# A three-stage attention-and-experts kernel: the two small score stages of neighbouring units put into common steps, and both units prepared one tile ahead

## The reference, cut to what matters

```python
def _attn_ref(q, k, v, alpha):                   # q, k, v, alpha: (4, 8, 768, 48)
    state = np.zeros((B, H, D, D))
    for t in range(S):
        state = alpha[:, :, t, :, None] * state + np.einsum('bhd,bhe->bhde', k[:, :, t], v[:, :, t])
        y[:, :, t] = np.einsum('bhd,bhde->bhe', q[:, :, t], state)
    return y

def _moe_ref(x, w_in, w_out):                    # x: (3072, 384), d_ff 2048
    h = x @ w_in
    g = np.where(h > 0.0, h, np.exp(np.minimum(h, 0.0)) - 1.0)
    return g @ w_out

def _moe2_ref(x, domain_probs, w1, w2):          # 4 experts, 1024 wide
    p = domain_probs / (domain_probs.sum(-1, keepdims=True) + 1e-09)
    for e in range(E):
        out += p[:, e:e + 1] * (np.maximum(x @ w1[e], 0.0) @ w2[e])
    return out

# reference: y = attention; x = y as (3072 tokens, 384); moe2(moe(x))
```

## Time and profile before

| what | value |
|---|---|
| time, median of 3 runs | 1290.7 us |
| the profiled execution, its time and its span | 1291.18 us, 1289.4 us |
| TensorE (PE) busy | 1276.2 us, 99% of the span |
| VectorE (DVE) busy | 849.3 us, 66% |
| ScalarE (ACT) busy | 631.6 us, 49% |
| GpSimd (POOL) busy | 500.3 us, 39% |
| granted TensorE clock | full in all 40 slices |

### The profile page before, as it was taken

How to read it: one execution, slowest core, us unless ns; L and a number is a source line. 1 busy time by engine, 2 the same in 40 slices (tenths; PEclk the granted TensorE clock), 3 DMA queues, 4 the chain that set the end, 5 groups by cost and what they waited for, 6 DMA issues and landing times.

```text
span 1289.4 us, 24688 instructions
## 1 busy us (share of the span) xinstructions
PE 1276.2 (99%) x9681; PEld 1055.8 (82%) x9681; DVE 849.3 (66%) x1245; ACT 631.6 (49%) x1051; POOL 500.3 (39%) x416
## 2 busy tenths in 40 slices
PE   7999999999999999999999999999999999999999
PEld 7888888888888888888888888888888888888887
DVE  8777868665676765676766567676567555654445
ACT  2766444367434357634436743435763444653332
POOL 2147959510476720084752056671009300000011
PEclk9999999999999999999999999999999999999999
DMA  4354635463445245436336344534543333523330
GB/s 174 105 200 131 191 120 167 128 176 108 163 147 164 87 116 167 142 130 208 103 107 175 123 141 149 158 99 129 153 161 111 98 100 98 156 86 111 98 98 26
DMA packets 84343, 170.92 MB, mean 133 GB/s; under 512 B 29186, under 2 KB 30722, under 8 KB 84228
## 3 DMA queue, kind: packets, MB, share of 16 engines
q1 hardware_dynamic: 83936, 169.21, 42.6%
q10 hardware_dynamic: 292, 0.14, 0.0%
HBM read 163.24 MB, written 6.08 MB: 131 GB/s over the span
## 4 chain that ended last, share of the span: by engine, by line
PE 97%; DVE 1%; issue 0%; DMA 0%; ACT 0%; SPq 0%; DVEq 0%; ACTq 0%
PE ps_o L699 16%; PE ps_h L699 15%; PE ps_o L701 15%; PE ps_o L700 15%; PE ps_h L701 15%; PE ps_h L700 15%; PE ps_att L677 1%; PE ps_att L603 1%; PE ps_att L635 1%; PE ps_att L520 1%; PE ps_att L534 1%; DMA alpha<-in_a 0%; DVE k_level L835 0%; DVE q_low L834 0%; DVE blocks L858 0%
## 5 line engine op out<-in xcount | busy, mean ns | idle before, releaser
L899 DVE TENSOR_TENSOR w_lo<-w_stage,w_hi 128x768 fp32r<-128x768 f32 x288 | 332.5, 1155 | 33.9 <-ACT w_hi L1125 30.5
L699 PE MATMUL ps_o<-g_hi,w_lo 128*128 128x512 f32 x864 | 341.1, 395 | 0.0
L701 PE MATMUL ps_o<-g_hi,w_hi 128*128 128x512 f32 x864 | 336.5, 389 | 0.0
L700 PE MATMUL ps_o<-g_lo,w_hi 128*128 128x512 f32 x864 | 336.4, 389 | 0.0
L699 PE MATMUL ps_h<-x_hi,w_lo 128*128 128x512 f32 (+1 forms) x861 | 335.3, 389 | 0.2 <-DVE x_lo L939 0.2
L701 PE MATMUL ps_h<-x_hi,w_hi 128*128 128x512 f32 (+1 forms) x861 | 334.5, 389 | 0.0
L700 PE MATMUL ps_h<-x_lo,w_hi 128*128 128x512 f32 (+1 forms) x861 | 334.5, 389 | 0.0
L1156 ACT ACTIVATE g_hi<-ps_h 128x512 fp32r<-128x512 f32 x184 | 110.0, 598 | 432.3 <-PE ps_h L701 432.3
L919 DVE SCALAR_TENSOR_TENSOR g_lo<-ps_h,g_hi 128x512 fp32r<-128x512 f32 x184 | 126.7, 689 | 207.9 <-ACT g_hi L1156 207.8
L1125 ACT CAST w_hi<-w_stage 128x768 fp32r<-128x768 f32 x288 | 239.3, 832 | 8.6 <-DMA w_stage<-in_w 7.3
L330 POOL TENSOR_TENSOR products<-blocks 128x384 f32<-128x384 f32 x150 | 191.4, 1295 | 94.3 <-DMA blocks<-in_a_blocks 71.5
(11 more groups left out here) (115 smaller groups left out, 943.9 us busy)
## 6 DMA issues: line engine op xcount, KB each, us to landing
w_stage<-in_w SPq DMA_DIRECT2D x288, 384.0 KB, 3.2
k_level<-in_k SPq DMA_DIRECT2D x12, 512.0 KB, 6.1
q_low<-in_q SPq DMA_DIRECT2D x12, 512.0 KB, 6.9
alpha<-in_a SPq DMA_DIRECT2D x12, 512.0 KB, 4.0
v_tok<-in_v SPq DMA_DIRECT2D x12, 512.0 KB, 4.5
p_rows<-p_norm SPq DMA_DIRECT2D x6, 1024.0 KB, 9.0
values_states<-in_v_heads SPq DMA_DIRECT2D x20, 256.0 KB, 4.6
out<-acc SPq DMA_DIRECT2D x18, 256.0 KB, 4.3
```

The lines of the kernel that those rows point to most:

```text
L699: nc.tensor.matmul(dst, lhs[1], rhs[0], start=first, stop=False)
L700: nc.tensor.matmul(dst, lhs[0], rhs[1], start=False, stop=False)
L701: return nc.tensor.matmul(dst, lhs[0], rhs[0], start=False, stop=last)
L899: nc.vector.tensor_tensor(wl[n % WRING][:], stage[n % STAGE][:], wh[n % WRING][:].bitcast(F32), ALU.subtract).then_inc(w_low, 1)
```

## The change: what it does

1. **Common pieces.** Both units of a tile begin their pieces at the same step (4; in tile 0, 15), and `PIECES` is now a pair of tables, one for even and one for odd units. Levels 16 and 32 of the odd unit fall into the same steps as those of the even one (piece 0 and 2). The later pieces of the odd unit come at 13, 15 and 23. In level 16 and 32 the even unit uses the left half of the bank and the odd unit the right half (`level_bank`).
2. **Put aside.** ScalarE copies the odd unit's scores from PSUM to `scores_aside` (`set_aside`, three copies of 128x256), and places them from there when the even unit's attention is done.
3. **Both units prepared ahead.** The odd unit's `unit`, `blocks`, `low` and `block` jobs move from steps 12 to 28 of its own tile into the tile in front. `PARTS_AT` has three columns now: tile 0, tile 1, and tiles 2 and up.
4. **Waits.** `bank_free` is replaced by functions that name the reader of each bank. The load of the queries waits for the placing of those of two units back.
5. **Last sums.** The last two steps' outputs are made sum by sum, the third in two halves of 256 tokens in the `ps_att` banks, and added and stored in four parts (`LAST_SUMS`, `last_outputs`, `add_last`).

```diff
-PIECES = {0: ("L", LOW), 2: ("L", LOW + 1), 4: ("K", 0), 6: ("KV", 0), 11: ("Y", 0)}
-BANK_AT = {("L", LOW): 0, ("L", LOW + 1): 2, ("K", 0): 3, ("KV", 0): 5, ("Y", 0): 7}
-STATES_AT = {6: (0,), 7: (1, 2), 10: (3,)}
-X_AT = {11: 0, 12: 1}
+PIECES = ({0: ("L", LOW), 2: ("L", LOW + 1), 4: ("K", 0), 6: ("KV", 0), 11: ("Y", 0)},
+          {0: ("L", LOW), 2: ("L", LOW + 1), 13: ("K", 0), 15: ("KV", 0), 23: ("Y", 0)})
+BANK_AT = {("L", LOW): (0, 0), ("L", LOW + 1): (2, 2), ("K", 0): (3, 9), ("KV", 0): (5, 11), ("Y", 0): (7, 13)}
+STATES_AT = ({6: (0,), 7: (1, 2), 10: (3,)}, {15: (0,), 16: (1, 2), 18: (3,)})
+X_AT = ({11: 0, 12: 1}, {23: 0, 24: 1})
...
     at = PARTS_AT[kind][min(tile, 2)][v]
...
 PARTS_AT = {
-    "unit": ((2, 12), (-STEPS + 26, 12)),
-    "blocks": ((8, 19), (-STEPS + 29, 15)),
+    "unit": ((2, 3), (-STEPS + 26, -STEPS + 35), (-STEPS + 24, -STEPS + 34)),
+    "blocks": ((8, 19), (-STEPS + 29, -STEPS + 40), (-STEPS + 17, -STEPS + 28)),
...
-    "low": ((5, 20), (-STEPS + 33, 18)),
-    "block": ((10, 23), (-STEPS + 35, 18)),
-    "place": ((22, 35), (-STEPS + 46, 31)),
-    "piece": ((15, 28), (4, 28)),
+    "low": ((5, 9), (-STEPS + 33, -STEPS + 42), (-STEPS + 30, -STEPS + 42)),
+    "block": ((10, 23), (-STEPS + 33, -STEPS + 42), (-STEPS + 19, -STEPS + 32)),
+    "place": ((22, 34), (-STEPS + 46, 18), (-STEPS + 31, 17)),
+    "piece": ((15, 15), (4, 4), (4, 4)),
 }
...
+LAST_SUMS = [(m, slice(0, TILE)) for m in range(KT - 1)] + [(KT - 1, slice(TILE // 2 * i, TILE // 2 * (i + 1))) for i in range(2)]
...
         def level_bank(u, l, sd):
-            return bank(NBANK * (u - LEAD) + BANK_AT["L", l] + (sd if l == LOW else 0))
+            width = SPANS * PAIRS * COL // 2
+            return bank(BANK_AT["L", l][u % 2] + (sd if l == LOW else 0))[:, width * (u % 2):width * (u % 2 + 1)]
...
+            def set_aside(u, l, sd):
+                act.wait_ge(step_done, pair(u, l))
+                if u > LEAD + 1:
+                    act.wait_ge(rect, 2 * lev(u - 2, LEVELS - 1))
+                nc.scalar.copy(scores_aside[:, 2 * (l - LOW) + sd, :], level_bank(u, l, sd)).then_inc(put_aside, 1)
...
+            def keys_free(u, c):
+                if u % 2 == 0:
+                    pe.wait_ge(rect, 2 * lev(u, LOW) - 1 + c)
+                    pe.wait_ge(put_aside, aside(u, c))
+                elif c == 0:
+                    pe.wait_ge(st_ready, states_before(u - 1, SPANS))
+                else:
+                    pe.wait_ge(xa_ready, 2 * (u - 1) + 1 - EARLY)
...
+            def last_outputs():
+                pe.wait_ge(xa_ready, 2 * UNITS - EARLY)
+                for k, (m, cols) in enumerate(LAST_SUMS):
+                    for n in (ALL - 2, ALL - 1):
+                        pe.wait_ge(g_ready, n + 1)
+                        last = products(last_sum(k), [w[n % WRING][:, MODEL + m * P:MODEL + (m + 1) * P] for w in (wh, wl)],
+                                        [g[n % GS][:, cols] for g in (gh, gl)], m == KT - 1 and n == ALL - 2, n == ALL - 1)
...
             def add_last(t):
+                added = (EXPERTS - 1) * KT * t + (EXPERTS - 2) * KT
+                dve.wait_ge(acc_added, added)
+                dve.wait_ge(o_step, ALL - 2)
+                nc.vector.tensor_tensor(acc[:, KT - 1, :], ps_o[KT - 1][:], acc[:, KT - 1, :], ALU.add).then_inc(acc_added, 1)
+                for n, (m, cols) in enumerate(LAST_SUMS):
...
+                    nc.vector.tensor_tensor(acc[:, m, cols], last_sum(n), acc[:, m, cols], ALU.add).then_inc(acc_added, 1)
```

More of the change, by code:

```diff
@@ L82, in step_of @@
     tile, v = divmod(u - 2, 2)
-    at = PARTS_AT[kind][min(tile, 1)][v]
+    at = PARTS_AT[kind][min(tile, 2)][v]
     return None if at is None else STEPS * tile + at
@@ L444, in store @@
             def store(t):
-                for m in range(KT):
-                    sp.wait_ge(acc_added, (EXPERTS - 1) * KT * t + (EXPERTS - 2) * KT + m + 1)
-                    sp.dma_start(out[m][:, t * TILE:(t + 1) * TILE], acc[:, m, :]).then_inc(stored, 16)
+                parts = LAST_SUMS if t == TILES - 1 else [(m, slice(0, TILE)) for m in range(KT)]
+                for n, (m, cols) in enumerate(parts):
+                    sp.wait_ge(acc_added, (EXPERTS - 1) * KT * t + (EXPERTS - 2) * KT + n + 1 + (t == TILES - 1))
+                    sp.dma_start(out[m][:, t * TILE + cols.start:t * TILE + cols.stop], acc[:, m, cols]).then_inc(stored, 16)
             load_early(0)
@@ L624, in outer @@
                 s = u % 2
-                for side in range(2):
-                    bank_free(u, BANK_AT["KV", 0] + side)
+                kv_free(u)
                 pe.wait_ge(v_in[s], 16 * (u // 2 + 1))
@@ L667, in attend @@
                 pe.wait_ge(vs_ready, 2 * (u - LEAD + 1))
-                for span in range(2):
-                    bank_free(u, BANK_AT["Y", 0] + span)
+                outputs_free(u)
                 for c in range(2):
@@ L682, in attention @@
             def attention(kind, u, i):
-                if kind != "piece" or i not in PIECES:
+                if kind != "piece" or i not in PIECES[u % 2]:
                     return
-                kind, l = PIECES[i]
+                kind, l = PIECES[u % 2][i]
                 if kind == "L":
-                    for i in range(2 if l == LOW else 1):
-                        bank_free(u, BANK_AT[kind, l] + i)
+                    levels_free(u, l)
                     pairs(u, l)
@@ L736, in output @@
                     last = products(ps_o[m][:], [w[n % WRING][:, MODEL + m * P:MODEL + (m + 1) * P] for w in (wh, wl)],
[L737 removed]
+                                    [g[n % GS][:] for g in (gh, gl)], f == 0, f == nf - 1 or (n == ALL - 3 and m == KT - 1))
                     if f == nf - 1 and m < KT - 1:
@@ L780, in _ @@
                     attention(*event)
-                output(J)
+                if J < ALL - 2:
+                    output(J)
+            last_outputs()
         @block.vector
@@ L1044, in attention @@
                 if kind == "piece":
-                    if i in PLACES_AT:
-                        what, l, sd = PLACES_AT[i]
+                    for what, l, sd in PLACES_AT[u % 2].get(i, ()):
                         if what == "level":
                             place(u, l, sd)
+                        elif what == "aside":
+                            set_aside(u, l, sd)
                         elif what == "queries":
@@ L1234, in attention @@
                     block_ops(u, i)
-                elif kind == "piece" and i in PIECES:
-                    kind, l = PIECES[i]
+                elif kind == "piece" and i in PIECES[u % 2]:
+                    kind, l = PIECES[u % 2][i]
                     if kind == "L":
```

124 lines of the change are left out of this document (74 added, 50 removed).

## The result

| | before | after |
|---|---|---|
| median | 1290.73 us (1290.49 to 1291.43, 5 runs) | 1305.07 us (1302.57 to 1306.22, 5 runs) |
| profiled execution, its span | 1291.18, 1289.4 us | 1302.57, 1300.8 us |

By the two medians the change costs 14.3 us, where 13.8 were forecast. The ratio of the runs, with its 95% interval, is 1.0103 [1.0092, 1.0114], which is 11.9 to 14.7 us: slower, clear of the noise. The profiled execution of after is the shortest of its five. From the first `output` matmul (57.27 before, 55.94 after) to the end of the span its trace has 12.7 us more, and that is what can be read.

What follows compares the result with a forecast made beforehand. TensorE, busy 99% of the span, was taken to bound the kernel. Losses of 16.0 + 0.8 + 0.9 = 17.7 us against gains of 3.3 + 0.6 = 3.9 gave +13.8, so 1304.5 us; range 1295 to 1313.

Steps and rivals of the forecast that it cites:

- Common pieces: Levels 16 and 32: merging two units' pieces saves the fixed 0.34 and 0.33 us, in five tiles 3.3 us.
- Last sums: End of the program: last addition 0.27 us shorter, last store 0.3 us less, 0.6 us gained in sum.
- Step 40, stall 5.1: End of tile 0: TensorE's sum 2, ready at 231.4, waits for `weigh` until 236.53, 5.1 us lost.
- Step 48, stall 10.9: End of tile 0: TensorE's sum 2, ready at 269.1, waits for `weigh` until 280.0, 10.9 us lost.
- The two places, 234.47 and 277.9: When GpSimd, with more preparation queued ahead, begins `add_part` of steps 40 and 48 in tile 0.
- late by less than the stall and need not add to it: `lower_elu` and `lower_w` behind VectorE, and weight loads behind SyncE's wait for products, add no loss of their own.
- Steps 10 to 16, 0.8: Tile 0: query multiplications and GpSimd's decay delay `lower_elu`, which TensorE needs; 0.8 us lost, between 0 and 2.
- Later tiles, 0.9 lost: Tiles 1 to 3: the odd unit's products around both `add_part`s cost 0 to 1 us each, 0.9 together.
- Rival 2: GpSimd runs near its best, stretches at 0.81 of the time: 1291.5 us, halfway to the forecast 1298; chance 0.15.
- The upper bound: VectorE's added work makes GpSimd's stretches in tile 0 10% longer: 6.2 us more, 22.2 us in all.
- Rival 1: GpSimd's lateness in tile 0 is absorbed, only the gains are left: 1287 to 1288 us; chance 0.07.
- rival 3: The 5.1 us delay of step 40's `add_part` comes back in tiles 1 to 3 too: 1319 us; chance 0.08.

Runs made afterwards that it cites:

- e6_pieces_apart: e5_later_still with the two units' level pieces apart again, the even unit's before the step's hidden states, the odd unit's after; 1291.42 us, 1.0002 of before.
- e5_later_still: The changed kernel with preparation and pieces later: tile 0's pieces at step 18, tile 1's at 15, unit 5's blocks loaded after tile 0; 1289.06 us, 0.9981 of before.
- e3_three_parts: The changed kernel with a third buffer for the weighed parts, so `weigh` no longer waits for its own step's addition; 1305.82 us, 1.0111 of before.
- e9_preparation_back: e5_later_still with the preparation of units 4 and 5 put back in steps 33 to 52, as in the changed kernel; 1305.25 us, 1.0104 of before.
- e7_blocks_by_gpsimd: The changed kernel with the block loads of units 4 and 5 issued from GpSimd's queue instead of SyncE's; 1307.97 us, 1.0132 of before.
- e2_half_products: The changed kernel with GpSimd's 30 products of units 4 and 5 computed over half their columns; 1298.68 us, 1.0063 of before.
- e8_waits_alone: The kernel before with six waits for small loads put in for TensorE, at steps 20 and 44 of tiles 1 to 3; 1313.35 us, 1.0172 of before.

## Why the prediction was right, point by point

- **Common pieces, 3.3 gained.** 0.34 at level 16; at level 32 305.89 - 303.95 - 0.45 = 1.49 for both, where two took 2 x 0.89: 0.29. 5 x 0.63 = 3.2, and e6_pieces_apart gives 2.4 by the times. Right.
- **Last sums, 0.6.** 0.5 from the start of the last outputs to the end; the store's part is 0.2 (2.1 to 1.9) and not 0.3.
- **Step 40, stall 5.1.** 4.6 lost, of which only 2.9 is wait and 1.7 slow clock. `add_part` came 0.8 us later than forecast, but TensorE was ready for sum 2 at 234.51 and not at 231.4, for it had lost time at steps 10 to 13, 33 and 38 (3.9 us, and its first `output` had come 1.3 us earlier than before): 5.1 + 0.8 - 3.1 = 2.8.
- **Step 48, stall 10.9.** 7.0 lost, of which 5.2 is the first wait and most of the rest slow clock. The place was forecast to 1.1 us (sum 2 at 278.93, not 280.0). The stall is smaller since TensorE came late: GpSimd's time is given, and what TensorE loses on the way isn't lost again at that wait. The way it took was partly another (the reduction in front of `weigh`, not the addition).
- **The two places, 234.47 and 277.9.** They came at 235.26 and 276.81, but each by two misses that cancelled. The first product of unit 4 began at 207.55 and not at 204.98, and GpSimd's work from there to the addition took 27.7 us and not 29.5. The first of unit 5 began at 253.86 and not at 252.5, and the work from there took 22.9 us and not 25.4.
- **Not in the forecast.** 1.1 us for late weights at 211 us and 1.2 us for the scores' placement at step 38: "late by less than the stall and need not add to it" was wrong in kind. They came before the stalls and so made them shorter. And the clock.
- **Steps 10 to 16, 0.8.** 1.6: gaps of 1.07 and 0.56 at 110.05 and 112.80, both for `g_lo` as forecast; within 0 to 2.
- **Later tiles, 0.9 lost.** None. From one tile's level 16 piece to the next, 207.43 us between tiles 2 and 3 where it was 208.12: 0.7 less, the merges alone.

The sum of what the trace names is 4.6 + 7.0 + 1.6 + 1.1 + 1.2 - 3.2 - 0.5 = 11.8 us of the 12.7. Most of the other 0.9 lies in small distances: 0.3 at 264 us, 0.2 at 345 us, and the first matmul behind each short wait, 0.34 from start to start instead of 0.227. The 1.6 us by which the median run of after is longer than the profiled one have no trace.

So the kernel lost its time at the two forecast places and by the forecast queue of GpSimd, but that the sum came out this near is in part luck. The two stalls together cost 11.6 us and not 16.0, and some 3.3 of the 11.6 are the slow clock, which the forecast hadn't. Losses at steps 10 to 16, at 211 us and at step 38 that were forecast too small or at nothing filled 3.1 of the gap.

Rival 2, GpSimd near its best, put its stretches at 0.81 of the forecast's time. They took 0.94 and 0.90, so the truth lies between, nearer to the forecast. The upper bound, VectorE disturbing GpSimd more than before, didn't come at all: a product of units 4 and 5 took 1.23 and 1.24 us in the mean, and 1.30 and 1.29 before. Rival 1 fails on the times, rival 3 on the later tiles.

## What to carry to other kernels

When a helper engine works in order for two masters, count what a moved job puts ahead of the short instruction that someone waits for, from the last time the helper is known to be free (here a load's landing) to that instruction. Such a chain gave two places within 1.1 us here, though its parts were each off by 1.4 to 2.6 us. Moving the jobs to where their results are needed, and not as early as possible, kept the gain and removed the loss (e5_later_still, 0.9981). And an in-order consumer in between passes lateness on by whichever of its instructions is next, so that taking away one handshake bought nothing here (e3_three_parts).

## What the runs showed of the hardware

A wait of TensorE costs more than its length. Behind the first `output` there are 13 waits of 2.5 us and more in the traces of six of these kernels. After 12 of them some 6 to 12 matmuls of 512 columns start 0.427 us apart instead of 0.227, the 1.2 GHz level instead of the 2.4: 1.5 to 1.8 us in all behind ten of them, and 2 and 2.4 us behind two of those of 5 us (e9_preparation_back, e3_three_parts). After one of 3.10 us (e7_blocks_by_gpsimd) they don't. The slow starts begin at once behind the three waits of 5 us and the one of 3.91 (e3_three_parts), and 0.2 to 1.5 us later behind the others. Of two waits of 2.0 to 2.1 us one was followed by it, and so was the one of 1.80 us among small matmuls (e2_half_products); of those up to 1.65 us (e8_waits_alone) none. The Trainium skill (TensorE: Matmul & The Clock Gate, HAM oscillation — how this bites in real kernels) describes a kernel whose waits for data send the array back to the lower clock again and again. The traces agree in kind: the windows of after at a granted clock of 0.60 and 0.53, and of e8_waits_alone at 0.64, each stand right behind such a wait.
